# Attention and MLP on one core: the small token block moved to the front of the MLP, its x prepared on POOL, and two projections at each block border

## The reference: what is computed

```python
x = attn_out.transpose(0, 2, 1, 3).reshape(2304, 512)
h = x @ w_in                         # 512 -> 2048
sp = where(h > 20, h, log1p(exp(min(h, 20))))
y = (h * tanh(sp)) @ w_out           # 2048 -> 512
```

## Time and profile before

| | us |
|---|---|
| three runs | 662.26 median (661.83 to 662.86) |
| the profiled execution | 663.03 |
| its span in the profile | 661.2 |
| PE busy | 624.7 (94%) |
| ACT busy | 431.1 (65%) |
| DVE busy | 334.7 (51%) |
| POOL busy | 259.3 (39%) |
| chain that ended last | PE 85%, POOL 6%, DMA 3% |

### The profile page before, as it was taken

The page is one execution under the profiler, slowest core; times in us unless marked ns, Lnnn a source line. Parts: engine busy times, 40 slices in busy tenths (PEclk is TensorE's granted clock), DMA queues, the critical chain, the costliest instruction groups (busy, mean ns, idle before and its releaser), DMA issues.

```text
span 661.2 us, 12740 instructions
## 1 busy us (share of the span) xinstructions
PE 624.7 (94%) x4562; PEld 478.2 (72%) x4562; DVE 334.7 (51%) x577; ACT 431.1 (65%) x691; POOL 259.3 (39%) x214
## 2 busy tenths in 40 slices
PE   2899999999998988999899999899999899999998
PEld 1666666666665556888688888688887788888996
DVE  3777768777787653535523333343334333334331
ACT  2777878778776737857448575476756476665763
POOL 3868777769677176336820000520004200003000
PEclk9999999999999999999989999899999899999999
DMA  6667656676675824000041000311000210000010
GB/s 204 187 220 235 204 168 217 201 231 189 185 206 150 233 56 111 1 0 1 0 128 63 1 1 1 105 22 63 0 0 0 63 63 0 0 0 1 11 54 33
DMA packets 38608, 59.63 MB, mean 90 GB/s; under 512 B 4240, under 2 KB 23824, under 8 KB 38576
## 3 DMA queue, kind: packets, MB, share of 16 engines
q1 hardware_dynamic: 38576, 59.20, 30.1%
HBM read 42.60 MB, written 9.51 MB: 79 GB/s over the span
## 4 chain that ended last, share of the span: by engine, by line
PE 85%; POOL 6%; DMA 3%; issue 2%; DVE 1%; SPq 1%; ACT 1%; POOLq 0%; DVEq 0%; ACTq 0%
PE ps_s L615 12%; PE ps_s L567 11%; PE ps_h L686 10%; PE ps_h L688 10%; PE ps_h L687 10%; PE ps_y L703 9%; PE ps_y L704 9%; PE ps_y L705 9%; PE ps_t L594 6%; POOL xb_l L502 3%; POOL xb_h L500 2%; DMA v_st<-v_in 1%; DMA raw<-qk_in 1%; PE ps_t L604 1%; DVE xb_l L992 1%
## 5 line engine op out<-in xcount | busy, mean ns | idle before, releaser
L686 PE MATMUL ps_h<-xb_h,win_hi 128*128 128x512 f32 (+1 forms) x320 | 121.5, 380 | 10.2 <-POOL xb_l L502 8.9
L894 DVE TENSOR_SCALAR_CACHE_REDUCE minus_s<-ps_s 128x576 f32<-128x576 f32 x144 | 106.1, 753 | 39.5 <-PE ps_s L567 38.8
L688 PE MATMUL ps_h<-xb_h,win_lo 128*128 128x512 f32 (+1 forms) x320 | 120.2, 376 | 0.0
L687 PE MATMUL ps_h<-xb_l,win_hi 128*128 128x512 f32 (+1 forms) x320 | 119.8, 374 | 0.0
L762 ACT ACTIVATE prob<-minus_s,neg_max 128x576 f32<-128x576 f32 x128 | 97.9, 768 | 32.8 <-DVE minus_s L894 32.7
L965 DVE TENSOR_TENSOR h_sb<-h_sb,m_sb 128x1024 f32<-128x1024 f32 x36 | 51.4, 1426 | 133.5 <-ACT m_sb L825 133.5
L814 ACT ACTIVATE h_sb<-ps_h 128x512 f32<-128x512 f32 x72 | 42.8, 597 | 110.7 <-PE ps_h L688 110.7
L703 PE MATMUL ps_y<-wout_hi,gh 128*128 128x512 f32 x288 | 112.8, 392 | 2.3 <-issue 2.3
L567 PE MATMUL ps_s<-qk_b,qk_a 64*128 64x288 f32 (+1 forms) x320 | 100.0, 440 | 14.8 <-DMA qk_b<-qk_a 11.6
L705 PE MATMUL ps_y<-wout_hi,gl 128*128 128x512 f32 x288 | 112.8, 392 | 0.0
L704 PE MATMUL ps_y<-wout_lo,gh 128*128 128x512 f32 x288 | 112.7, 391 | 0.0
(11 more groups left out here) (48 smaller groups left out, 940.2 us busy)
## 6 DMA issues: line engine op xcount, KB each, us to landing
raw<-qk_in SPq DMA_DIRECT2D x32, 576.0 KB, 4.2
v_st<-v_in SPq DMA_DIRECT2D x32, 160.0 KB, 2.5
qk_b<-qk_a SPq DMA_DIRECT2D x32, 144.0 KB, 2.5
x_transposed<-xt SPq DMA_DIRECT2D x64, 72.0 KB, 3.1
y_out<-y_mem SPq DMA_DIRECT2D x18, 256.0 KB, 2.1
win_raw<-w_in SPq DMA_DIRECT2D x16, 256.0 KB, 4.4
wout_raw<-w_out SPq DMA_DIRECT2D x16, 256.0 KB, 4.4
x_raw<-x_transposed SPq DMA_DIRECT2D x4, 1024.0 KB, 5.7
```

What stands on the lines that cost most here:

```text
L686: nc.tensor.matmul(o, wh, x_h, start=(k == 0), stop=False)
L687: nc.tensor.matmul(o, wh, x_l, start=False, stop=False)
L688: mm = nc.tensor.matmul(o, wl, x_h, start=False, stop=(k == KC - 1))
L894: nc.vector.tensor_scalar(minus_s[:, ring(word)], ps_s[:, score_buf(word, m), :, 0:SIDE], -1.0, None, ALU.mult, ALU.min, accum_out=neg_max ...
```

## The change

- The block of 256 tokens becomes block 0; blocks 1 to 4 have 512 tokens. Block 0 has 4 chunks with slots 1, 2, 0, 1 of the g buffers.
- `load_x(0)` and `load_r(0)`, at their old place in SP's order, move 256 tokens instead of 512. They go to halves of `x_raw`; the high and low parts of block 0 lie in `x_rec`. The reciprocals of block 1 are loaded into `xb_l`, later ones into `x_rec`.
- POOL scales and splits the x of block 0 in three instructions of 128x1024, after its step 15 and ahead of step 16, which holds the last `split_w_in`. ACT and DVE no longer split x.
- ACT and DVE split tiles 0 to 3 of w_out instead, at the place where they split x. POOL splits tiles 4 to 11 without waits for PE, then x of block 1 (without a wait for `h_done`), then tiles 12 to 15.
- PE's order: the last `project` of a block now stands between `hidden(b, 0)` and `hidden(b, 1)` of the next, the one ahead of it ends its own block, and nothing stands between `hidden(b, 1)` and `hidden(b, 2)`.
- ACT takes y tiles 0 and 1 after chunk 0's tanh, 2 and 3 within chunk 1 (it was one chunk later for each). The last block now has 4 y tiles.
- DVE's order of `multiply`, `cap` of the next chunk and `split_g` is as before.

```diff
 # PE
-            for c in range(CHUNKS):
-                hidden(0, c)
-                if c == 2:
-                    pe.wait_ge(rt_taken, 6)
-                if c >= 2:
-                    project(0, c - 2)
-            with pe.Fori(1, NB - 1) as b:
-                one_block(b)
-            one_block(NB - 1)
-            for c in range(chunks_of(NB - 1) - 2, chunks_of(NB - 1)):
-                project(NB - 1, c)
+            pe.wait_ge(first_split, 1)
+            hidden(0, 0)
+            hidden(0, 1)
+            hidden(0, 2)
+            pe.wait_ge(rt_taken, 6)
+            project(0, 0)
+            hidden(0, 3)
+            project(0, 1)
+            project(0, 2)
+            one_block(1, 3)
+            with pe.Fori(2, NB) as b:
+                one_block(b, 7)
+            project(NB - 1, 7)
...
+            def one_block(b, last):
+                hidden(b, 0)
+                project(b - 1, last)
+                hidden(b, 1)
+                for c in range(2, 8):
+                    hidden(b, c)
+                    project(b, c - 2)
+                project(b, 6)
...
             def project(b, c):
-                w, n = tokens_of(b), FT // chunks_of(b)
-                pe.wait_ge(g_split, CHUNKS * b + c + 1)
-                if isinstance(b, int) and b == 0:
-                    pe.wait_ge(w_out_split, n * (c + 1))
+                w, n, slot = tokens_of(b), FT // chunks_of(b), g_slot(b, c)
+                pe.wait_ge(g_split, chunks_until(b) + c + 1)
+                if small(b):
+                    if c == 0:
+                        pe.wait_ge(w_first, W_FIRST)
+                    else:
+                        pe.wait_ge(w_out_split, n * (c + 1) - W_FIRST)
 # POOL
+            def split_first_x():
+                scale_x(0)
+                nc.gpsimd.tensor_scalar(first_h[:], x_first[:], 1.0, 1.0, ALU.mult, ALU.mult).then_inc(first_hi, 1)
+                pool.wait_ge(first_hi, 1)
+                nc.gpsimd.tensor_tensor(first_l[:], x_first[:], first_h[:].bitcast(F32),
+                                        ALU.subtract).then_inc(first_split, 1)
...
             step(15, 1)
-            scale_x(0)
+            split_first_x()
             step(16, 0)
...
-            for c in range(FT):
-                if c >= 4 and c % 2 == 0:
-                    pool.wait_ge(h_done, c)
+            for c in range(W_FIRST, 12):
                 split_w_out(c)
-            for b in range(1, NB):
+            split_x(1)
+            for c in range(12, FT):
+                split_w_out(c)
+            for b in range(2, NB):
                 split_x(b)
 # ACT
-            act.wait_ge(x_scaled, 1)
-            for k in range(KC):
-                nc.scalar.activation(xb_h[:, k, :], x_raw[:, k, :], ACT.Copy).then_inc(first_hi, 1)
             act.wait_ge(rt_done, 6)
-            one_block(0)
+            act.wait_ge(w_out_loaded, 16 * FT)
+            for c in range(W_FIRST):
+                nc.scalar.activation(wout_hi[:, c, :], wout_raw[:, c, :], ACT.Copy).then_inc(w_first_hi, 1)
+            one_block(0, 0)
 # DVE
-            for k in range(KC):
-                dve.wait_ge(first_hi, k + 1)
-                nc.vector.tensor_tensor(xb_l[:, k, :], x_raw[:, k, :], xb_h[:, k, :].bitcast(F32),
-                                        ALU.subtract).then_inc(first_split, 1)
+            for c in range(W_FIRST):
+                dve.wait_ge(w_first_hi, c + 1)
+                nc.vector.tensor_tensor(wout_lo[:, c, :], wout_raw[:, c, :], wout_hi[:, c, :].bitcast(F32),
+                                        ALU.subtract).then_inc(w_first, 1)
             take_reciprocals(1)
             cap(0, 0)
...
-            def one_block(b):
+            def one_block(b, more):
                 for c in range(chunks_of(b)):
                     multiply(b, c)
                     if c < chunks_of(b) - 1:
                         cap(b, c + 1)
-                    elif not isinstance(b, int) or b < NB - 1:
+                    elif more:
                         cap(b + 1, 0)
                     split_g(b, c)
 # SP
             def load_r(b):
-                x_free(b)
+                if b == 1:
+                    for e in range(2):
+                        sp.wait_ge(pv_done[e], PAIRS)
+                elif b > 1:
+                    sp.wait_ge(h_done, units_until(1))
+                    sp.wait_ge(xb_split, KC * (b - 1))
+                dst = (r_first, second_rec)[b] if b < 2 else x_rec
```

More of the change, by code:

```diff
@@ L70, with small, first_token, chunks_until @@
 FT = DF // P
-UNITS = 16
-CHUNKS = 8
+W_FIRST = 4
+SMALL = TOKENS - (NB - 1) * TB
 G_SLOT = (0, 1, 2, 0, 1, 2, 0, 1)
+G_SLOT_SMALL = (1, 2, 0, 1)
+def small(b):
+    return isinstance(b, int) and b == 0
 def tokens_of(b):
-    return TB if not isinstance(b, int) or b < NB - 1 else TOKENS - (NB - 1) * TB
+    return SMALL if small(b) else TB
+def first_token(b):
+    return 0 if small(b) else TB * b - (TB - SMALL)
 def chunks_of(b):
[L83 to L90, removed]
+    return 4 if small(b) else 8
+def chunks_until(b):
+    return 0 if small(b) else 8 * b - 4
+def units_until(b):
+    return 2 * chunks_until(b)
+def projections_until(b):
+    return 0 if small(b) else 7 * b - 4
+def tiles_until(b):
+    return 0 if small(b) else 4 * b - 2
+def g_slot(b, c):
+    return G_SLOT_SMALL[c] if small(b) else G_SLOT[c]
 def due(value):
@@ L270, in attention_mlp @@
         gl = sb2("gl", [P, 3, 1024], F32R)
+        second_rec = xb_l.bitcast(F32)
         ps_h = top.enter_context(nc.psum_tensor("ps_h", [P, 4, 512], F32))
@@ L678, in hidden @@
                         for k in range(KC):
-                            if f == 0:
-                                if isinstance(b, int) and b == 0:
-                                    pe.wait_ge(first_split, k + 1)
-                                else:
-                                    pe.wait_ge(xb_split, KC * (b - 1) + k + 1)
+                            if f == 0 and not small(b):
+                                pe.wait_ge(xb_split, KC * (b - 1) + k + 1)
                             wh, wl = win_hi[:, k, f * P:f * P + P], win_lo[:, k, f * P:f * P + P]
-                            x_h, x_l = xb_h[:, k, 0:w], xb_l[:, k, 0:w]
@@ new lines, in project @@
+                pe.wait_ge(g_split, chunks_until(b) + c + 1)
[4 more added lines that the diff above has]
+                        pe.wait_ge(w_out_split, n * (c + 1) - W_FIRST)
+                for t in range(w // P):
+                    if c == 0 and not small(b):
+                        if isinstance(b, int) and b == 1:
+                            if t < SMALL // P:
+                                pe.wait_ge(y_taken, t + 1)
+                        else:
+                            pe.wait_ge(y_taken, tiles_until(b) - 4 + t + 1)
@@ L834, in one_block @@
                 for c in range(chunks_of(b)):
                     take_h(b, 2 * c)
-                    if c == 2 and due(b):
-                        take_y(b - 1, 2)
-                        take_y(b - 1, 3)
+                    if c == 1:
+                        for t in range(2, tiles):
+                            take_y(b - 1, t)
                     take_h(b, 2 * c + 1)
                     tanh_softplus(b, c)
-                    if c == 1 and due(b):
-                        take_y(b - 1, 0)
-                        take_y(b - 1, 1)
+                    if c == 0:
+                        for t in range(min(2, tiles)):
+                            take_y(b - 1, t)
@@ L852, in _ @@
+            one_block(0, 0)
             act.wait_ge(r_stored, 64 * BATCHES)
[L853 to L856, removed]
+            one_block(1, SMALL // P)
+            with act.Fori(2, NB) as b:
+                one_block(b, 4)
+            for t in range(4):
                 take_y(NB - 1, t)
@@ L998, in _ @@
             dve.wait_ge(r_stored, 64 * (EARLY // PB))
[L999 to L1002, removed]
+            one_block(0, True)
+            one_block(1, True)
+            with dve.Fori(2, NB - 1) as b:
+                one_block(b, True)
+            one_block(NB - 1, False)
 def rope_table():
```

111 lines of the change are left out of this document (54 added, 57 removed).

## The result

The change makes the kernel slower: 667.12 us median against 661.46 of the kernel before, ratio 1.0085 (95% interval 1.0061 to 1.0109), where 1.0035 was forecast. A second measurement of the same two kernels gave 666.16 against 662.26, ratio 1.0056 (1.0034 to 1.0078). The two profiled executions differ by less: span 664.2 against 661.2.

A forecast was written before the change was run, and what follows sets the result against it. PE was busy 94% of the span, so only its waits and half clock could move. Terms of -2.05, -1.75, -1.45, +1.8, +5.0, +0.5 and +0.3 gave +2.35 on 662.26: 664.6 us, range 660.5 to 669.3 (the forecast's own 661.5 to 667.5).

The forecast's parts named there:

- earlier start of `hidden(0, 0)`: MLP start: PE starts at 239.8 in place of 241.87, -2.05 us in all with the v tile.
- waits in the first unit: Block 0's first unit in the MLP: the waits for the x split go, -1.75 us.
- `project(0, 0)`: Block 0's first projection: gap of 1.8 for g plus 0.8 for the clock, 2.7 lost in place of 4.15, -1.45 us.
- `project(0, 2)`: Block 0, right behind project(0, 1): g of chunk 2 late, gap 1.4 and 0.4 for the clock, +1.8 us (0 to 3.5).
- borders, with the extra of block 1: Four borders: gap 3.49, 5.5 us each, 22.0 against 16.96, +5.0; DVE's cap waiting for POOL into block 1, +0.5.
- end (PE's last matmul to the span's end): Kernel end: four y tiles in place of two, tile 3 waiting for tile 1's store, +0.3 us (0 to 1).
- Rival D: Block 0: POOL's unbroken work slows DVE, Exp to Exp 10.9, g of chunk 2 3.7 later, +4.5: 669; chance 0.12.
- The v tile: End of attention: half the x load ahead of it, so PE's 1.54 us wait goes, -1.5 (bounds -1.54 and 0).
- A: Borders: the gap doesn't open, borders cost nothing, 664.6 - 22.5 = 642 us; chance 0.04.
- B: Borders: the gap opens but the clock holds, four times 1.9 less, 657.0 us; chance 0.09.
- C: Borders: two stretches of half clock at each, +6.0, 670.6 us; chance 0.11.

The follow-up runs named there:

- dve_order: The changed kernel, but at a block's end DVE splits g of the last chunk before it caps chunk 0 of the next block: 646.51 us, ratio 0.9755.
- pe_order: The changed kernel, but PE runs hidden(b, 1) ahead of the last projection of the block before; DVE's order stays: 645.62 us, ratio 0.9733.
- filled: The changed kernel with 14 useless matmuls of 512 columns between hidden(b, 0) and the last projection of the block before: 660.20 us, ratio 0.9963.
- pool_pause: dve_order, but POOL stops before w_out's tile 9 until g of chunk 0 is split: 647.78 us, ratio 0.9769.
- late_low: dve_order, but DVE takes the reciprocals and caps chunk 0 before splitting the four low parts of w_out's first tiles: 644.40 us, ratio 0.9735.
- after_again: The changed kernel once more, no edit, with its own profile, beside the kernel before: 666.16 us, ratio 1.0056.
- old_border: The changed kernel with one projection behind each of hidden(b, 0) and hidden(b, 1) again, ACT's take_y one chunk later: 659.89 us, ratio 0.9952.
- spread: late_low, but PE runs hidden(0, 3) ahead of project(0, 0) and hidden(1, 0) ahead of project(0, 2): 643.08 us, ratio 0.9690.

## Why the prediction was right, and where its sizes were off

The direction and the mechanism at the borders were right, the size was too small: 1.0035 forecast, 1.0085 and 1.0056 measured; 667.12 lies in the range. By the steps, from the first profile of each kernel:

| step | forecast | measured |
|---|---|---|
| earlier start of `hidden(0, 0)` | -2.05 | -1.30 (241.87 to 240.57) |
| waits in the first unit | -1.75 | -1.75 |
| `project(0, 0)` | 2.7 lost, -1.45 | 5.8 lost, +1.65 |
| `project(0, 2)` | +1.8 | +0.1 |
| borders, with the extra of block 1 | 22.5 lost, +5.5 | 21.3 lost, +4.3 |
| end (PE's last matmul to the span's end) | +0.3 | 0.0 (3.58 and 3.56) |
| sum | +2.35 | +3.0 |

That the two sums lie so close is in part luck: `project(0, 0)` cost 3.1 us more than forecast and the start brought 0.75 less, while `project(0, 2)` cost 1.7, the borders 1.2 and the end 0.3 less.

- *Borders:* right, and shown twice: dve_order and pe_order take them away from two sides. The gap was forecast as 3.49 and is 3.44 (3.67 less 0.23); at the border into block 1 it is 4.08, the extra being the cap beside POOL's scaling, as forecast. The clock was taken as 1.9 a border, 7.6 in all; the trace gives 6.9 (21.3 less 14.4 of idle time), of which filled wins back 6.0.
- *`project(0, 0)`* is the term that was mis-sized. DVE's work was priced from rows of the kernel before, where it met less of POOL's. There the low parts of x took 4.42 us, and the cast of chunk 0 started in a pause of POOL (259.56 to 260.19):

```profile
241.03 4.42 DVE L992 TENSOR_TENSOR xb_l<-x_raw,xb_h 128x512 fp32r<-128x512 f32 x4 [0.25 <-ACT xb_h L849]
...
260.04 0.68 DVE L977 CAST gh<-h_sb 128x1024 fp32r<-128x1024 f32 x1
```

In the changed kernel the four low parts of w_out took 5.12, began 1.1 after PE's first `hidden` where 0.7 was forecast, and the cap behind them took 1.54 in place of 1.18, so Exp started 9.1 after PE and not 7.9. From there to g it took 12.35 and not 11.18, mostly because the cast took 1.10 and the low part 2.16 in place of 1.52. pool_pause shows that POOL's work lengthens this second part (3.70 in place of 6.42); that it is also what lengthens the low parts of w_out and the cap is likely, but no run shows it. late_low takes 2.0 of the gap away, pool_pause 2.7. Rival D had this mechanism but put it at chunk 2; Exp to Exp was 9.17 and 9.77 (249.66, 258.83, 268.60), not its 10.9.
- *`project(0, 2)`:* g of chunk 2 was 3.3 later than forecast (280.29, not 277.0), but behind the late first projection PE asked for it only at 280.4; in late_low the gap is there, 2.6.
- *The v tile:* its wait went as forecast. None of the eleven profiles with the load of 256 tokens shows it, and all three with the old load do (1.5, 1.7 and 1.7 us).
- *Rivals.* A is out. B's claim that the clock may hold came true at single places (border into block 1 in after_again), not at all four. C was not seen at any of the 12 borders of the three profiles; 6.8 us of half clock did come behind `project(0, 0)`, in after_again, dve_order, pe_order and old_border.

The profiles don't settle the size. From PE's first `hidden` to the span's end it is 419.3 and 416.7 us before, 423.6, 422.4 and 423.8 after, so 5.3 more in the mean, and the earlier start gives 1.3 back, or 2.4 without what the first pairs of heads differed by (PE's first reciprocals at 201.61 before and 202.68 after): 3 to 4 us. That is the 3.7 us by which the kernels differ in the second measurement and 1.7 to 2.7 short of the 5.7 in the first. The attention part varies by over 2 us between executions of the same kernel, and two profiles of one kernel and three of the other can't close that; the rest stays open.

## What to carry to other kernels

When work is reordered to hide one latency, list for each instruction what it waits for through every in-order engine, not only its operands: here the last projection waited for the next block's matmuls because the cap of that block stood ahead of a split on DVE. Moving that cap behind the split turned a loss of 0.6 to 0.9% into a gain of 2.5%, and the kernel before gets 2.3% from the same step and the two projections at the border, without the rest of the change. A gap on PE costs more than its length where half clock follows it; matmuls of no use in the gap bought that part back.

## What the runs showed of the hardware

- The same gap does not always have the same clock behind it. Idle 2.28 and 2.27 us at the same place of the kernel before: half clock for 3.4 us in one execution, none in the other. Behind the 4.0 us ahead of `project(0, 0)`, in seven profiles with that gap, it lasted 3.4 us three times and 6.8 us four times. Gaps of 3.3 to 4.0 us: a fall at 11 of the 12 borders in three profiles of the changed kernel; the one without had 3.28. A gap of 2.0 in late_low had no fall, one of 1.9 in spread had one. The Trainium skill, "TensorE: Matmul & The Clock Gate", section "Why this matters for your kernels", puts the limit at gaps of about 3 us; here gaps of 2 us are already in doubt.
- A DVE cast or multiplication from SBUF to SBUF waited for the whole POOL instruction that came first: a cast of 0.69 us took 5.11 (269.88 to 274.99) beside a POOL instruction of 5.07 (269.37 to 274.44). The other way round POOL's instructions grew too: a tile of w_out took 2.0 us beside an idle DVE and up to 3.3 beside a busy one (253.62 to 256.90 in late_low). Four POOL instructions in place of one let DVE in between them (its multiplication took 2.12 and not 4.20, POOL's four 6.49 and not 4.62). That is the lock of the Trainium skill's "SBUF — State Buffer", section "Who interferes with whom", and the runs agree with it.
